# Two products of a bilinear block by seven block products in place of eight, on nine tiles of 484 tokens

## The reference

```python
def _moe_ref(x, w_in, w_out):          # first block, d_ff 2048
    h = np.maximum(x @ w_in, 0.0)
    return h * h @ w_out

def _moe2_ref(x, w1, w2, w3, w_out):   # second block, d_ff 1024
    a = x @ w1
    b = x @ w2
    h = a * b @ w3
    return h @ w_out
```

## Time and profile before

| | |
|---|---|
| median of 3 runs | 1292.43 us (1292.36 to 1293.12) |
| profiled execution, its own time | 1292.21 us |
| its span, first to last instruction | 1290.6 us |
| PE busy | 1265.6 us (98%) |
| DVE, ACT, POOL busy | 592.3, 487.0, 19.4 us |

### The profile page before, as it was taken

How to read it: one execution, slowest core, us unless ns; L and a number is a source line. 1 busy time by engine, 2 the same in 40 slices (tenths; PEclk the granted TensorE clock), 3 DMA queues, 4 the chain that set the end, 5 groups by cost and what they waited for, 6 DMA issues and landing times.

```text
span 1290.6 us, 15958 instructions
## 1 busy us (share of the span) xinstructions
PE 1265.6 (98%) x5977; PEld 1049.3 (81%) x5977; DVE 592.3 (46%) x974; ACT 487.0 (38%) x897; POOL 19.4 (2%) x35
## 2 busy tenths in 40 slices
PE   8979999999999999999999999999999999999996
PEld 6657888888888888888889988888888888888886
DVE  6666876665665757565546432222222222222121
ACT  6565564544554545544445322212121212121111
POOL 1000000000000000000000000000000000000000
PEclk9998999999999999999999999999999999999999
DMA  9986441121222221221224321101000010000000
GB/s 295 364 293 215 133 134 59 58 90 58 89 66 88 62 96 53 73 70 53 90 74 148 99 66 50 33 33 32 34 26 39 24 41 12 37 0 33 1 34 17
DMA packets 49815, 105.49 MB, mean 82 GB/s; under 512 B 4072, under 2 KB 5096, under 8 KB 48744
## 3 DMA queue, kind: packets, MB, share of 16 engines
q1 hardware_dynamic: 45464, 84.43, 20.1%
q0 software_dynamic: 4304, 20.45, 4.2%
HBM read 68.16 MB, written 36.70 MB: 81 GB/s over the span
## 4 chain that ended last, share of the span: by engine, by line
PE 95%; DMA 3%; DVE 1%; ACT 0%; issue 0%; SPq 0%; DVEq 0%; ACTq 0%; POOLq 0%
PE ps_y L528 47%; PE ps_h L528 29%; PE ps_t L528 17%; DMA g_scratch<-g_extra 1%; DMA wp_scratch<-stage 1%; DMA g_scratch<-stage 1%; PE ps_t L587 1%; PE ps_h L587 0%; PE ps_t L552 0%; DMA raw<-in_moe_w_in 0%; DVE v_lo L1002 0%; ACT v_hi L799 0%; DVE t L1002 0%; DVE X_lo L1002 0%; DVE stage L1113 0%
## 5 line engine op out<-in xcount | busy, mean ns | idle before, releaser
L528 PE MATMUL ps_y<-v_hi,X_hi 128*128 128x512 f32 (+1 forms) x576 | 219.6, 381 | 2.2 <-DVE stage L1091 2.2
L1002 DVE TENSOR_TENSOR t<-t,ps_t 128x512 f32<-128x512 f32 (+1 forms) x72 | 47.4, 658 | 373.9 <-ACT t L799 373.9
L528 PE MATMUL ps_y<-v_lo,X_hi 128*128 128x512 f32 (+1 forms) x576 | 218.1, 379 | 0.0
L528 PE MATMUL ps_y<-v_hi,X_lo 128*128 128x512 f32 (+1 forms) x576 | 218.0, 378 | 0.0
L1002 DVE TENSOR_TENSOR v_lo<-t,v_hi 128x512 fp32r<-128x512 f32 (+1 forms) x216 | 143.1, 662 | 155.4 <-ACT v_hi L799 155.4
L799 ACT CAST v_hi<-t 128x512 fp32r<-128x512 f32 (+1 forms) x216 | 129.0, 597 | 197.5 <-DVE t L1002 197.5
L799 ACT COPY t<-ps_h 128x512 f32<-128x512 f32 (+2 forms) x78 | 46.6, 598 | 383.9 <-PE ps_t L528 380.9
L885 ACT ACTIVATE t<-ps_h 128x512 f32<-128x512 f32 (+1 forms) x144 | 82.6, 574 | 155.2 <-PE ps_h L528 154.7
L1002 DVE TENSOR_TENSOR t<-t 128x512 f32<-128x512 f32 (+1 forms) x144 | 94.9, 659 | 97.6 <-ACT t L885 96.7
L528 PEld LDWEIGHTS ps_y<-v_hi,X_hi 128*128 128x128 f32 x576 | 108.8, 189 | 22.0 <-issue 2.6
L528 PEld LDWEIGHTS ps_y<-v_hi,X_lo 128*128 128x128 f32 x576 | 108.8, 189 | 20.4
(11 more groups left out here) (157 smaller groups left out, 1872.6 us busy)
## 6 DMA issues: line engine op xcount, KB each, us to landing
raw<-g_scratch SPq DMA_DIRECT2D x64, 256.0 KB
raw<-in_moe_w_in SPq DMA_DIRECT2D x32, 256.0 KB
raw<-in_x_T SPq DMA_DIRECT2D x32, 256.0 KB
raw<-in_x_tok SPq DMA_DIRECT2D x32, 256.0 KB
y_scratch<-stage POOLq DMA_DIRECT2D x8, 1024.0 KB, 6.0
raw<-y_scratch SPq DMA_DIRECT2D x32, 256.0 KB
out<-stage POOLq DMA_DIRECT2D x8, 1024.0 KB, 4.2
g_scratch<-g_extra SPq DMA_DIRECT2D x14, 512.0 KB, 6.9
```

The lines of the kernel that those rows point to most:

```text
L528: mm = nc.tensor.matmul(dst, w, m, start=first and n == 0, stop=last and n == 2)
L1002: return nc.vector.tensor_tensor(dst, a, b, op)
```

## The change

The first block is untouched. In the second, a and b of one tile are taken as the two block rows of one product: the weights are a 2 x 2 block matrix (w1 and w2 by the two halves of K), the tokens another (halves of K by two groups of 242 tokens). Seven products of sums of blocks replace the eight: A11, S2, S3, S1, A12, A22, S4 on the side of the weights, and B11, T2, T3, T1, B21, T4, B22 on the side of the tokens. Each is of 128 columns of weights and 242 of tokens with two K pieces and the three passes, so 6 matmuls; a chunk has 42. Nine tiles of 484 tokens cover the 4352 (the last one begins 4 tokens early).

- GpSimd makes S1 to S4 for four groups g (two halves of d_ff by two K pieces): four `tensor_tensor` of 128x512 each, in a chain. ACT and DVE split all 28 results (`S_round`, `S_lower`) in the state tile's slots 4 to 11 for g = 0, 1 and within the first three chunks of tile 0 for g = 2, 3.
- DVE makes T1 to T4 for each tile (`T_sums`) and, with ACT, splits the seven token operands (`set_round`, `set_lower`), in chunk 7 of the tile before. The operands have one set of buffers; operand j is refilled when product j of chunk 7 is over.
- The seven products of a chunk fill four banks, so the next chunk's products wait until DVE has multiplied the last one's (`ab_done`). Product 5 shares a bank with product 1 and waits for ACT's copy of that (`P1_copied`). DVE joins the products with five additions and two multiplications.
- The output is made transposed: wp is the stationary operand, v the moving one, 12 matmuls of 484 columns. It is stored as 512 x 4352 and turned back on the host.
- The ring of prefetched pieces ends at state slot 2; w1, w2, wp and the tokens are loaded by other DMAs after it. The y buffer is laid out anew. The scratch of the software DMA is set to 4096 bytes.

```diff
+            def load_S(g):
+                half, kk = g // 2, g % 2
+                blocks = [(moe2_w1, kk), (moe2_w1, 2 + kk), (moe2_w2, kk), (moe2_w2, 2 + kk)]
+                for dst, (w, c) in zip(S_raw(g), blocks):
+                    sp.dma_start(dst, w[c * P:(c + 1) * P, half * C:(half + 1) * C]).then_inc(S_loaded[g], 16)
...
+            sp.wait_ge(piece_split, N_RING)
+            load_S(0)
+            load_S(1)
...
+            def S_sum(g):
...
+                A11, A12, A21, A22 = S_raw(g)
+                S2, S3, S4 = S_sums(g)
+                pool.wait_ge(S_loaded[g], 16 * 4)
+                step(S3, A11, A21, ALU.subtract)
+                pool.wait_ge(S_summed, 4 * g + 1)
+                step(A21, A21, A22, ALU.add)
+                pool.wait_ge(S_summed, 4 * g + 2)
+                step(S2, A21, A11, ALU.subtract)
+                pool.wait_ge(S_summed, 4 * g + 3)
+                step(S4, A12, S2, ALU.subtract)
...
+            pool.wait_ge(y_stored, 16 * NB)
+            S_sum(0)
+            pool.wait_ge(S_split, N_SETS)
+            S_sum(1)
             store_y(SR, NT)
+            pool.wait_ge(set_ready, N_SETS)
+            S_sum(2)
+            pool.wait_ge(S_split, 3 * N_SETS)
+            S_sum(3)
...
+            def ab_chunk(t, m):
+                chunk = KG * t + m
+                wait_for(pe, ab_done, chunk)
                 cols = slice(m % 4 * P, (m % 4 + 1) * P)
+                for j, dst in enumerate(places):
+                    if m == 0:
+                        pe.wait_ge(set_ready, N_SETS * t + j + 1)
+                    if isinstance(t, int) and t == 0 and m == 4:
+                        pe.wait_ge(S_split, 3 * N_SETS + j + 1)
+                    if j == 4:
+                        pe.wait_ge(P1_copied, chunk + 1)
+                    for kk in range(2):
+                        g = m // 4 * 2 + kk
+                        mm = product(dst, S_hi[g][j][:, cols], S_lo[g][j][:, cols], B_hi[:, j, kk], B_lo[:, j, kk],
+                                     kk == 0, kk == 1)
+                    mm.then_inc(prod_done, 1)
```

The DVE's side of a chunk, whose steps the prediction counts:

```diff
+                tt(u2, P1, bank_X[:, 0:HT], ALU.add).then_inc(u2_done, 1)
...
+                tt(u34.rearrange("p (s n) -> p s n", s=2), bank_Y[:, 0:TT].rearrange("p (s n) -> p s n", s=2),
+                   u2.unsqueeze(1).to_broadcast([P, 2, HT]), ALU.add).then_inc(u34_done, 1)
...
+                tt(c22, u34[:, 0:HT], bank_Y[:, HT:TT], ALU.add).then_inc(c22_done, 1)
...
+                tt(c11, P1, bank_W[:, HT:TT], ALU.add).then_inc(c11_done, 1)
...
+                tt(c21_12, u34, bank_Z[:, 0:TT], ALU.add).then_inc(c_done, 1)
...
+                tt(vv[:, 0:HT], c21_12[:, 0:HT], c11, ALU.mult)
+                tt(vv[:, HT:TT], c21_12[:, HT:TT], c22, ALU.mult).then_inc(ab_done, 1)
```

More of the change, by code:

```diff
@@ L56, in build_program @@
     WARM = 9
+    RAW_AT = 4736
     RAW = 8
@@ L470, in _ @@
[L470 to L473, removed]
+            sp.wait_ge(set_ready, N_SETS)
+            load_y(y_tiles[1])
+            sp.wait_ge(wp_split, KG)
+            load_S(2)
+            sp.wait_ge(y_stored, 16 * (NB + 1))
+            load_S(3)
@@ L944, in second_block, with ab_chunk @@
-            def second_block(t, n, chunk, then):
-                for m in range(1, KG):
-                    chunk(m)
-                then(0)
+            def ab_chunk(t, m, refill=True):
+                chunk = KG * t + m
+                act.wait_ge(prod_done, N_SETS * chunk + 1)
+                wait_for(act, ab_done, chunk)
+                copy(P1, bank_W[:, 0:HT]).then_inc(P1_copied, 1)
+                if m == KG - 1 and refill:
+                    for j in range(N_SETS):
+                        set_round(t + 1, j)
+                wait_for(act, out_acc, chunk - 1)
+                act.wait_ge(ab_done, chunk + 1)
+                copy(v_hi[:, m % 2, 0:TT], vv).then_inc(ab_hi, 1)
+                if isinstance(t, int) and t == 0 and m:
+                    for g, j in S_chunks.get(m, []):
+                        S_round(g, j)
@@ L948, in second_block, with drain_out @@
+            def drain_out(t):
                 act.wait_ge(out_acc, KG * t + KG)
                 wait_for(act, out_stored, t * 16)
+                for o in (0, 2):
+                    copy(stage[:, o, 0:TT], ps_y[:, o, 0:TT]).then_inc(out_drained_act, 1)
+            def second_block(t, last=False):
+                for m in range(1, KG):
+                    ab_chunk(t, m, not last)
+                if not last:
+                    ab_chunk(t + 1, 0)
                 if isinstance(t, int) and t == 0:
-                    act.wait_ge(y_stored, 16 * (SR + 1))
@@ L952, in second_block @@
-                for r in range(0, n // P, 2):
-                    copy(stage[:, r, :], ps_y[:, r, :]).then_inc(out_drained_act, 1)
+                    act.wait_ge(S_split, 4 * N_SETS)
+                drain_out(t)
             act.wait_ge(g_stored[0], stored(0, LAST))
```

393 lines of the change are left out of this document (244 added, 149 removed).

## The result

The changed kernel took 1296.57 us, median of 8 runs (1294.49 to 1299.63), against 1292.46 (1292.11 to 1293.51) before: a ratio of 1.0033, 95% interval [1.0022, 1.0044]. It is slower by 4.1 us, where 1286.6 and faster were forecast. Its runs also spread over 5 us, where those of before keep within 1.4.

What follows compares the result with a forecast made beforehand. PE's instruction work was taken as the bound. From 1290.6 us, -25.2 matmul work, +19.7 handover waits, +2 slow clock and -2.3 end gave a 1284.8 us span; 1.6 and 0.2 more made 1286.6 us. Range 1276 to 1304.

Steps and rivals of the forecast that it cites:

- The products: Second block's matmuls: 114.2 ns at 242 columns, 215.0 at 484, 59.0 us a tile for nine tiles; gain 25.2 us.
- narrow forms: Rival: below a limit under 256 columns matmuls pay by the column, 195 ns at 242; 1531 us; chance 0.09.
- the line: Rival: columns / 2.4 + 13.3 ns fails, a matmul of 242 columns costs 120 ns; 1304 us; chance 0.07.
- The steady loop: Second block's chunks: DVE and ACT deliver before PE asks, with 0.7 us of slack at chunk 7; no cost.
- the rival that VectorE sets the pace: Rival: DVE delays PE by 1 us a tile at chunk 7, 8 us in all; 1295 us; chance 0.05.
- The end: After the last matmul: copies and one 1 MB store take 7.5 us where 9.8 stood; gain 2.3 us.
- Handover waits: State tile to second block's chunk 2: new PE waits behind loads, sums, splits and casts, 19.7 us.
- the entry: Start of second block, behind wp's splits: waits of 2.8 us at the first product and 1.1 at the fifth, 3.9.
- chunks 1 and 2: Second block's first tile: ACT's copy of product 1 stands behind casts awaiting GpSimd's sums; waits of 5.3 and 4.9 us.
- the state tile: Ahead of the second block: waits of 0.4 us at slot 4, 2.3 for g = 1's sums, 2.9 after slot 9; 5.6.
- I add 2 us: Handover: the clock at 0.50 after two or three long PE waits costs 2 us, 0 to 5.
- The dear handover: Rival: a GpSimd sum costs 1.6 us, waits and slow clock 27 + 5 us in place of 21.7; 1297 us; chance 0.17.

Runs made afterwards that it cites:

- run 1: Changed kernel with PE repeating matmuls in its waits (state tile's h chunks 6 and 15 twice more, fourth product of chunks 1 and 2 eight times more): 1295.46 us.
- run 2: Changed kernel with fewer repeats than run 1: h chunk 6 twice more, fourth product 8 and 4 times more in chunks 1 and 2: 1294.06 us.
- run 6: Changed kernel with wp loaded straight into the place of its low part, third group's loads ahead of wp's second half: 1295.41 us.
- Run 4: Changed kernel with the splits of the third and fourth weight groups one chunk later, at the ends of chunks 1 to 3: 1285.09 us.
- run 7: Changed kernel with the weight sums on VectorE instead of GpSimd, ahead of each group's first split: 1286.00 us.
- run 11: Changed kernel with the sums on VectorE and the third and fourth groups' splits later (run 7 and Run 4 together): 1284.82 us.

## Why the prediction was wrong

- **The products held.** 242 columns start 113 to 114 ns apart, as laid out; 484 columns start 219 apart where 215.0 was taken. Nine tiles at 59.15 us are 532.3 us against 556.5 by the starts measured before: a gain of 24.2 us where 25.2 was worked out. The rivals on narrow forms and on the line are out. This is 7% of the 371 us that a and b took and not an eighth: 3024 matmuls of 242 columns stand where 1536 of 512 and 192 of 256 stood, and each brings its 13.3 ns.
- **The steady loop costs nothing**: held. One wait of 0.27 us in 500; the rival that VectorE sets the pace is out.
- **The end** gained 2.7 us for 2.3.
- **Handover waits, 19.7 us**: in the ledger they came out at +19.7, and this is luck. The chains behind the waits are the ones that the prediction named, and the entry (3.55 for 3.9) and chunks 1 and 2 (6.0 for 5.3, 4.3 for 4.9) are near. But the state tile's 6.1 for 5.6 is made of 2.97 us at slot 4 where 0.4 was laid out, 1.15 at slot 8 for 2.3 and 1.97 after slot 9 for 2.9. And all are waits of a PE that had itself come later: the forecast's waits are those of a PE at full pace.
- **The step that failed is the handover's size, 19.7 us of waits plus "I add 2 us" for the slow clock.** The handover took 31 us (4.1 over before, plus 24.2 and 2.7 gained elsewhere), not 21.7. In the ledger the gap stands under the slow pace, 11.0 us for 2. But with the clock held up only 1 to 4 us came back (runs 1 and 2), within the 0 to 5 that the prediction gave it. So the term that was too small is the 19.7: the chains behind PE were later than laid out, and would have made PE wait some 27 to 30 us had it run at full pace (an estimate: 31 less 1 to 4). Three sizes in them were off. A group's first three GpSimd sums took 4.0 to 4.5 us, where 3.5 was laid out: 1.26 to 1.67 us a sum with starts 1.34 to 1.7 apart, for 1.15. The first loads let them start at 691.64 and not at 690.1 (the forecast's own terms give 689.7 for the landing, not 689.9). And ACT waited 0.78 and 1.29 us for loads of wp, which the sum didn't have at all (run 6: 1.2 us). VectorE lost 3.9 us beside the sums; turns were in the sum, so this was priced, if roughly. How the 7 to 10 us divide among these isn't shown.
- **The dear handover** (0.17; "1.6 us a sum, with turns, and 5 us of slow clock, 1297") is the rival that came in at its time, and its 27 + 5 us are close to what the handover took. Its price of 1.6 us a sum isn't what was measured: a group's four sums took 5.3 to 5.9 us, 1.33 to 1.47 each, around the 1.4 at which the prediction said that this rival begins. It had the same mechanism; only the sizes told the two apart, and no row of before had them. The nearest rows, a memset and an affine select, read one input or none, and I took a value worked out from the select, in the lower half of the bounds (0.52 to 1.91).
- **Not seen at all** was how cheap the cure is. The prediction took the order of splits as given. Run 4 shows that 11.5 us hung on splits standing in ACT's queue up to three chunks before anybody needs them, ahead of the copy that PE needs at once.

What stays open is the split among the causes to better than 2 or 3 us: kernels with long PE waits spread over 3 to 8 us from run to run, and the effects don't add up (runs 4, 7 and 11).

## What to carry to other kernels

A product count that falls by an eighth gives that much only where everything around it was waiting for the products. Count the preparation (sums, splits, loads) at the one place where nothing covers it, and put each piece into its engine's queue no earlier than its buffer or its reader asks for, behind what TensorE waits for now. Don't hand two-input arithmetic to GpSimd as if it were a free engine while VectorE works from SBUF: here 20 us of such GpSimd work, with nobody waiting for it, cost 7 us beside a VectorE that made the sums itself, and VectorE did the same sums in half the time. Where waits of one engine come out just as forecast but the total doesn't, look at when they happen and whether the parts agree too, and test a lower clock by filling the wait before putting the loss down to it.

## What the runs showed of the hardware

- With new weights for every matmul, TensorE's starts are 113.4 ns apart at 242 columns and 119.7 at 256, 219.4 at 484 and 226.8 at 512 (means over the second block, after and before): columns / 2.4 GHz + 13.3 ns within 1 ns, but for 484 columns, which take 4 ns more.
- A GpSimd addition of 128x512 takes 1.26 to 1.30 us alone and up to 1.67 beside VectorE; VectorE's 0.69 us for two inputs of SBUF becomes 1.0 to 1.8 (once 2.53, run 1), its 0.42 up to 1.48.
- In the changed kernel the granted clock fell to 0.50 at each wait of 2.56 us and more, and stood there for as long as 8 us (732 to 740) with PE busy 7.01 of 8.00. A wait of 1.97 us left it at 1.00 there (718 to 724), where one of 1.96 in run 1 was followed by 0.57 (720 to 724). With PE kept busy in the second block it stayed at 1.00. Its price in time was 1 to 4 us, because most of the time PE wasn't what was late.
